# Retention, routed experts and a rational layer on one core: new order of the last three token tiles, and transposes in place of identity products

## What is computed

```python
for t in range(S):                                   # per batch and head
    state = gamma * state + outer(k[t], v[t])
    y[t] = scale * q[t] @ state
x = y laid out as (B*S, H*D)                         # 1536 x 512

logits = x @ w_gate
e = argmax(logits)                                   # first expert among equals
gate_w = softmax(logits)[e]
# tokens go to their expert in order, up to capacity (384)
out[i] = gate_w[i] * (relu(disp[e] @ w1[e]) @ w2[e])[pos[i]]

h = out @ w_in                                       # 512 -> 2048
g = (a0 + a1*h + a2*h^2 + a3*h^3) / (1 + |b0||h| + |b1|h^2 + 1e-6)
result = g @ w_out                                   # 2048 -> 512
```

## Time and profile before

| | |
|---|---|
| median of 3 runs | 536.94 us |
| profiled execution, its own time | 536.65 us |
| span in the trace | 534.8 us |
| TensorE busy | 525.8 us, 98% |
| VectorE busy | 423.5 us, 79% |
| ScalarE busy | 329.6 us, 62% |
| Pool busy | 76.4 us, 14% |
| HBM read, written | 59.09 MB, 12.60 MB |

### The profile page before, as it was taken

The page is one execution under the profiler, slowest core; times in us unless marked ns, Lnnn a source line. Parts: engine busy times, 40 slices in busy tenths (PEclk is TensorE's granted clock), DMA queues, the critical chain, the costliest instruction groups (busy, mean ns, idle before and its releaser), DMA issues.

```text
span 534.8 us, 8739 instructions
## 1 busy us (share of the span) xinstructions
PE 525.8 (98%) x3209; PEld 439.0 (82%) x3209; DVE 423.5 (79%) x759; ACT 329.6 (62%) x508; POOL 76.4 (14%) x74
## 2 busy tenths in 40 slices
PE   6999999999999999999999999999999999999997
PEld 4888888888888888888788888888888888888885
DVE  2578788785856759577989999997888888787886
ACT  2464546584655747457969867658566566655652
POOL 3343342260101101003010010004000000200000
PEclk9999999999999999999999999999999999999999
DMA  9999959959968384903060000003000000200002
GB/s 194 232 247 254 275 199 392 396 147 389 380 237 303 149 332 144 398 29 99 23 217 1 1 21 20 1 1 113 7 21 20 1 0 1 80 1 0 0 1 79
DMA packets 65087, 72.26 MB, mean 135 GB/s; under 512 B 41234, under 2 KB 41746, under 8 KB 65044
## 3 DMA queue, kind: packets, MB, share of 16 engines
q1 hardware_dynamic: 58596, 57.96, 34.5%
q0 software_dynamic: 3136, 9.46, 5.2%
q10 hardware_dynamic: 3312, 4.28, 2.3%
HBM read 59.09 MB, written 12.60 MB: 134 GB/s over the span
## 4 chain that ended last, share of the span: by engine, by line
PE 96%; DMA 1%; DVE 1%; SPq 1%; issue 0%; ACT 0%
PE up_low L949 7%; PE up_low L950 7%; PE up_low L951 7%; PE bank L949 6%; PE bank L950 6%; PE bank L951 6%; PE up_high L955 6%; PE up_low L955 5%; PE yrows L949 4%; PE yrows L950 4%; PE up_high L951 4%; PE up_high L949 4%; PE up_high L950 4%; PE yrows L951 4%; PE up_high L956 3%; PE up_low L956 3%
## 5 line engine op out<-in xcount | busy, mean ns | idle before, releaser
L876 DVE TENSOR_TENSOR T<-raw,T 128x1024 fp32r<-128x1024 f32 x60 | 71.5, 1219 | 33.8 <-ACT T L870 33.8
L870 ACT ACTIVATE T<-raw 128x1024 fp32r<-128x1024 f32 x60 | 60.5, 1070 | 32.2 <-PE bank L951 31.8
L949 PE MATMUL up_low<-x2H,T 128*128 128x512 f32 x176 | 69.3, 394 | 0.0
L951 PE MATMUL up_low<-x2H,T 128*128 128x512 f32 x176 | 68.5, 389 | 0.0
L950 PE MATMUL up_low<-x2L,T 128*128 128x512 f32 x176 | 68.5, 389 | 0.0
L1529 ACT ACTIVATE sq<-up_low 128x512 f32<-128x512 f32 x44 | 26.2, 596 | 64.4 <-PE up_low L951 64.1
L1550 DVE SCALAR_TENSOR_TENSOR wa<-sq,coef,wa 128x512 f32<-128x512 f32 x48 | 35.9, 748 | 28.7 <-ACT wa L1531 28.7
L949 PE MATMUL bank<-T,hL 128*128 128x512 f32 x128 | 50.6, 395 | 0.0
L951 PE MATMUL bank<-T,hH 128*128 128x512 f32 x128 | 49.9, 390 | 0.0
L950 PE MATMUL bank<-T,hH 128*128 128x512 f32 x128 | 49.8, 389 | 0.0
L1543 ACT ACTIVATE rc<-wa,cst 128x512 f32<-128x512 f32 x48 | 34.8, 725 | 20.6 <-DVE wa L1550 15.9
(11 more groups left out here) (205 smaller groups left out, 1228.7 us busy)
## 6 DMA issues: line engine op xcount, KB each, us to landing
raw<-in_moe_w_dram SPq DMA_DIRECT2D x14, 2048.0 KB, 10.9
raw<-in_moe_w_dram SPq DMA_DIRECT2D x8, 512.0 KB, 5.1
w_out_raw<-in_moe_w_out_dram SPq DMA_DIRECT2D x4, 1024.0 KB, 17.1
ybuf<-ysb ACTq DMA_DIRECT2D x15, 256.0 KB
qin<-in_q_dram SPq DMA_DIRECT2D x12, 256.0 KB, 5.3
kin<-in_k_dram SPq DMA_DIRECT2D x12, 256.0 KB, 5.7
vin<-in_v_dram SPq DMA_DIRECT2D x12, 256.0 KB, 5.6
xbuf<-xt SPq DMA_DIRECT2D x12, 256.0 KB, 4.2
```

Source lines behind the costliest of these rows:

```text
L870: e.activation(W[w][:, 0, cols], raws[par][:, w, cols], ACT.Copy).then_inc(r.wH[w], 1)
L876: e.tensor_tensor(W[w][:, 1, cols], raws[par][:, w, cols], W[w][:, 0, cols].bitcast(F32), ALU.subtract).then_inc(r.wL[w], 1)
L949: nc.tensor.matmul(out_, aL, bH, start=start, stop=False)
L951: return nc.tensor.matmul(out_, aH, bH, start=False, stop=stop)
```

## The change

The eight products with the identity in `pe_x_stored` get the transpose flag; they still add into PSUM. In `pe_last_tiles`, `pe_values(11)` moves ahead of the logits of tile 10, the logits and rows of tile 11 move ahead of `pe_positions(10)` and of all `pe_x_late`, `pe_positions(11)` moves ahead of `pe_x_stored`, and `pe_index(9)` moves behind `pe_x_late(2)`. In `dve_last_tiles`, the copy of `lgT` of tile 11 moves ahead of `dve_place(10)`, and `dve_choose(11)` ahead of `dve_put(9)`. Pool does `pool_x_stored` ahead of all three `pool_low_rows`. ScalarE copies `xT` of tiles 10 and 11 before the rows of both.

```diff
@@ pe_x_stored
                 for s in range(NMAIN):
                     last = e.matmul(x_bank(kk)[:, s * P:(s + 1) * P], xd[:, s, kk * P:(kk + 1) * P], ident,
-                                    start=False, stop=False, skip_group_check=True)
+                                    is_transpose=True,                                    start=False, stop=False, skip_group_check=True)
             last.then_inc(main.xt, 1)
@@ pe_last_tiles
             t = NT - 1
             pe_query_state(t)
+            pe_values(t)
             pe_logits_apart(t - 1)
             pe_rows(t - 1)
             pe_logits_sum(t - 1)
-            pe_values(t)
+            pe_logits_apart(t)
+            pe_rows(t)
+            pe_positions(t - 1)
             pe_x_late(0, range(2))
-            pe_positions(t - 1)
-            pe_x_late(0, range(2, 3))
-            pe_logits_apart(t)
-            pe_x_late(0, range(3, KD))
-            pe_rows(t)
             pe_logits_sum(t)
+            pe_x_late(0, range(2, KD))
             pe_x_late(1, range(KD))
-            pe_index(t - 2)
+            pe_positions(t)
             pe_x_stored(range(2))
-            pe_positions(t)
             pe_x_stored(range(2, KD))
             pe_x_late(2, range(KD))
+            pe_index(t - 2)
             pe_index(t - 1)
@@ dve_last_tiles
             dve_choose(late + 1)
+            dve_logits_apart(late + 2)
             dve_place(late + 1)
             dve_fit(1)
             dve_count(late + 1)
-            dve_logits_apart(late + 2)
+            dve_choose(late + 2)
             dve_put(late)
-            dve_choose(late + 2)
             dve_lane(late + 1)
@@ the block of gpsimd
-            pool_low_rows(0)
             pool_x_stored()
-            for i in range(1, LAST):
+            for i in range(LAST):
                 pool_low_rows(i)
@@ the block of scalar
-            for t in range(NT):
+            for t in range(NT - 1):
                 act_tile(t)
-            act_evac_xT(NT - 1)
-            act_rows(NT - 1)
+            for t in range(NT - 2, NT):
+                act_evac_xT(t)
+            for t in range(NT - 2, NT):
+                act_rows(t)
             act_xH_first()
```

## The result

The changed kernel takes 538.72 us, median of 6 runs (537.54 to 539.74), against 536.86 (536.67 to 537.41) for the kernel before on the same chip: a ratio of 1.003, 95% interval 1.0017 to 1.0042. It is slower by about 1.9 us. The forecast was 536.6, with a range that ended at 537.2. The profiled execution took 539.41, its span is 537.6.

A forecast was written before the change was run, and what follows sets the result against it. TensorE, with 96% of the chain, was taken to bound the kernel. Of 1.1 us saved there, 0.3 to 0.4 reaches the second expert's gather: -0.35 us, 536.6 against 536.94, range 535.9 to 537.2.

The forecast's parts named there:

- What bounds the kernel: From 69 us to the expert loop: TensorE's lead is carried to the end, behind a 0.3 us wait for gathered rows.
- The 0.07 us between TensorE and DVE: Before x_late(2): fit(2) ends at 78.17, the weight load starts at 78.24, so shortening one engine alone gives almost nothing.
- Transposes: In x_stored: eight transposes take 0.9 us where eight products take 1.99, saving TensorE 1.1 us.
- values(11) first: TensorE, tiles 10 and 11: choose(10) starts at 72.85 instead of 71.89, costing tile 10 0.96 us.
- DVE: Choices of tiles 10 and 11: choose(11) starts at 74.93, fit(2) ends at 77.63 instead of 78.17, a lead of 0.55.
- Rival 5: DVE is stretched in the choice of tile 10 or 11: fit(2) 0.5 later, 536.9 to 537.1; chance 0.20 shared with others.
- Pool: x_stored ahead of low_rows(0): gathers run 69.3 to 71.7, low_rows(0) ends at 73.0 to 73.2, its readers covered.
- the 0.6 that I had given it: Slack in us between low_rows(0) ending at 73.0 to 73.2 and its readers, wanted at 73.7 and 74.0.
- TensorE behind that: After choose(11): x_late(2) starts at 77.65 instead of 78.24; half of the transposes' 1.1 us is idle before it.
- index(9) behind x_late(2): On DVE put(11) waits for index(9) until 78.95 instead of 78.53, leaving xL a lead of 0.3.
- Where the lead is cashed: At the second expert's gather: only the index's lead of 0.3 to 0.4 arrives; the rest becomes a longer wait.

The follow-up runs named there:

- e1: Kernel before with only the transpose flag on the eight products of x_stored, all orders kept; 537.02 us against 537.07 for the kernel before.
- e7: Kernel before with the transpose flag and inside in the tensor_scalar form that also gives its sum; 536.53 us against 537.16 for the kernel before.
- e5: Changed kernel with six products of zeros between rows(11) and positions(10), where TensorE idles; 538.53 us against 537.16 for the kernel before.
- e6: Changed kernel with each low_rows subtraction cut from 512 to 128 columns, part of the computation left out; 537.09 us against 537.16 for the kernel before.
- e2: Changed kernel without the transpose flag, x_stored as products again; 539.83 us against 537.07 for the kernel before.
- e8: Changed kernel with each low_rows subtraction in four pieces of 128 columns and index(9) ahead of positions(11); 539.14 us against 537.16 for the kernel before.
- e12: Changed kernel, unedited, measured again; 538.45 us against 536.81 for the kernel before.
- e4: Changed kernel with index(9) back in front of x_late(2), ahead of positions(11); 538.37 us against 537.07 for the kernel before.
- e10: Changed kernel with inside and hot_all in the tensor_scalar form that also gives its sum; 537.50 us against 536.81 for the kernel before.
- e11: Changed kernel with inside and hot_all in the form that gives its sum, and index(9) ahead of positions(11); 537.40 us against 536.81 for the kernel before.
- e9: Kernel before with inside in the form that gives its sum, without the transpose flag; 536.69 us against 536.81 for the kernel before.

## Why the prediction was wrong, point by point

*What bounds the kernel.* Right that the lead of TensorE before the loop is carried to the end, and that the gather of the second expert binds. The 0.07 us between TensorE and DVE is read rightly, but something is missing behind it: DVE's arrival was set by a third engine. TensorE's queue was full; fit(2) was held by low_rows(2) on Pool (e1, e7). The row was on the table, "inside" with 0.77 us, and I put most of it down to a wait for positions(11). A step that waits for a semaphore starts late; it doesn't last long. Its end at 77.65, 0.03 behind Pool's 76.35 + 1.27 = 77.62, was the sign:

```profile
76.35 1.27 POOL L893 TENSOR_TENSOR xtL<-xt,xtH 128x512 fp32r<-128x512 f32 x1 [2.23 <-ACT xtH L475]
```

*Transposes.* Right: eight in 0.86 us at full clock (e5, e6), not dearer than products. Their gain was nil on the order of before, because of the hold (e1); inside the changed kernel there is one (e2), of a size that the runs leave between 0.26 at the index and about a microsecond of the median.

*values(11) first.* Right: without holds choose(10) starts at 3.90 after index0 (e6: 74.38 - 70.48), predicted 3.95.

*DVE.* This is the step that failed: the sum for DVE takes every step at the time it has when nothing holds it, "inside" at 0.14 among them, and puts the holds by Pool at nothing. Predicted start of fit(2) 8.3 after index0; e6 shows 8.23 when nobody is held; the changed kernel has 9.75. The 1.5 us are the holds. Rival 5 named the mechanism, for one hold of 0.5 us and with a small part of 0.20; there were three, because the change puts Pool's three subtractions back to back just beside the chain.

*Pool.* I priced the move of low_rows by who reads xtL, and all of them were indeed covered. The first gather started 0.90 behind its index and not 0.24 (70.42 against 69.36 + 0.16), so low_rows(0) ended at 4.75 after index0 where 4.1 to 4.3 was forecast, inside the 0.6 that I had given it. I didn't price the move by who shares SBUF with it. The Trainium skill states the rule (SBUF — State Buffer, "Who interferes with whom"): a tensor_scalar of VectorE in a mode that uses both of its ports, or an operation with two inputs in SBUF beside one of Pool that reads SBUF, and an instruction of Pool take turns at a shared pair of ports, and whoever comes second stands still until the first is done. It names the form of tensor_scalar that writes its accumulator as exempt. Here inside (1.06), hot_all (0.54), fit (0.85) and cum (1.25) were held, and the accumulator's form was not (0.21 in e7): by that rule, the trace agrees. In e8 it doesn't wholly: "inside" was held past the ends of two pieces, to the end of the third, and the measurement decides. I should have weighed it as a rival by itself.

*TensorE behind that.* This is a second failure, of a term put at nothing. I foresaw about half a microsecond of idle time in front of x_late(2), and about 0.25 in front of positions(10) (73.7 to 73.95), and took idle time to cost only itself. The gap of 1.63 us in front of positions(10) was followed by 3.4 us at half clock, which cost 0.87 us at the index (e5). That is so in some executions: in the profiled ones of the changed kernel, e12 and e8, not in those of e2 and e4 with the same gap.

*index(9) behind x_late(2).* Right in kind: put(11) waits. In size 1.22 us with the low clock, 0.42 in e10 where 0.4 was forecast; 0.1 to 0.14 of it reaches the index (e11).

*Where the lead is cashed.* The wait for the rows grew, as foreseen, but with a delay and not with a lead. From index to turn it is 10.20 before, 10.69 after, 11.90 in e2, and 9.8 to 10.0 where TensorE doesn't wait (e6, e7, e11). What makes a gather land up to 1.7 us later is not settled; the weights' transfers of SyncE are beside it in all runs, and no run varied them. The forecast that they go out 1 us earlier was wrong, too: SyncE begins them 7.26 us after index0 (76.62), against 7.32 (76.22) before. The rows of x_stored landed 4.3 us after issue, at 76.2 us and not by 75, and SyncE waits for them.

*The sum of the loss.* At the index: order and flag without holds gain 12.12 - 11.64 = 0.48 (e6), the holds cost 13.07 - 11.64 = 1.43 (e5 against e6, both at full clock; the wait for index(9) shifts with them), and the low clock costs 13.94 - 13.07 = 0.87 (e5). That makes the 1.82 that the index is late. The later landing adds 0.49, and the end is 2.3 late. This is the sum of one profiled execution in which the clock fell; the medians differ by 1.6 to 1.9, and in the executions of e12 without a fall by 0.95.

## What to carry to other kernels

When work is moved on Pool, look at what VectorE does beside its new place, not only at who reads the result: small SBUF-to-SBUF steps in a chain of choices wait for a whole Pool instruction. The sign in a trace is a step that lasts several times its usual time and ends with Pool's instruction. Removing one held step passes the hold to the next one that is prone to it (e7, e10), so either free the whole chain or keep Pool out of its time; and cutting Pool's work into pieces doesn't do it (e8).

A saving on one engine is worth only what the last of all arrivals allows: the flag gave nothing alone, the form of inside nothing that stands out of the noise, and both together 0.6 us of the median (e1, e9, e7). No run has the new order with the whole chain free and nothing left out, so whether that order would then beat e7 is open.

## What the runs showed of the hardware

- A plain tensor_scalar of 128 x 3 values is held for as long as a 128 x 512 subtraction of Pool (1.06 us in place of 0.22), while one of 128 x 1 beside it isn't (lane_of, 0.27), nor the form with a sum (0.21).
- With the subtractions in pieces of 0.43 us, one behind the other on Pool, "inside" was held to the end of the third piece (1.06 us), while the later steps were held for less than a piece (0.56, 0.42 and 0.47 us; e8).
- After 1.6 us of idle weight loads in front of positions(10) the granted clock fell to 1.2 GHz for 3.4 us in the profiled executions of the changed kernel, e12 and e8, and stayed at 2.4 in those of e2 and e4, whose gap is the same, and of e11, where a gap of 1.60 us comes 2.8 us later (1 fall in its 12 executions). By the mean clocks it fell in 23 of 46 executions with the gap in front of positions(10), and in 6 of 44 with that gap at about half a microsecond or less. So the gap made the fall likelier and not certain; what else decides is open.
- The first gather for the second expert, issued while VectorE subtracts 128 x 1024 values from SBUF, took 1.80 us of Pool's time against 0.95 for the one behind it, in every kernel of this study (the earlier trace rows for the first). No run took the subtraction away, so that it is the cause is not shown.
